# Products of constants between TensorE's first products, and one TensorE program in place of two, with the last outputs turned among the experts' first blocks

## What is computed

```python
def _attn_ref(r, k, v, w, a, b):          # (4, 8, 768, 40) each
    state = zeros((B, H, D, D))
    for t in range(S):
        y[:, :, t] = einsum('bhd,bhde->bhe', rt, state)
        Sa = einsum('bhde,bhe->bhd', state, at)
        state = state * wt[:, :, None, :] - einsum('bhd,bhe->bhde', Sa, bt) \
            + einsum('bhd,bhe->bhde', vt, kt)
...
x = y as (4, 768, 320)
x = _moe_ref(x)      # gates, the best 2 of 4 experts; each expert: causal softmax attention of width 64, then wo
return _moe2_ref(x)  # relu(x @ w_in), halves u and v, v normalised, w_spatial @ v + b, (u * v) @ w_out
```

## Time and profile before

| what | us |
|---|---|
| three executions | 980.12, 989.87, 990.72 |
| median | 989.87 |
| the profiled execution | 986.48 |
| its span, first to last instruction | 984.6 |
| TensorE busy in it | 946.3 (96%) |
| VectorE, ScalarE, GpSimd busy | 490.4, 450.4, 265.8 |
| mean granted TensorE clock | 0.977 of full |

### The profile page before, as it was taken

One profiled execution on the slowest core, in us unless ns is written; L12 is line 12 of the kernel. 1 busy time (PEld: TensorE's weight loads), 2 busy tenths in 40 slices (PEclk: granted clock), 3 DMA queues, 4 the chain that ended last, 5 costly groups with the idle time before them and its releaser, 6 DMA issues.

```text
span 984.6 us, 36043 instructions
## 1 busy us (share of the span) xinstructions
PE 946.3 (96%) x15444; PEld 685.4 (70%) x15444; DVE 490.4 (50%) x1395; ACT 450.4 (46%) x1074; POOL 265.8 (27%) x442
## 2 busy tenths in 40 slices
PE   7899999999999999999998999999999999999998
PEld 4788888888888888876655655566555665556555
DVE  7677777777777777754055244421434214342120
ACT  6456565565565655653237234342343423434501
POOL 7434645545545545522200001100011000110021
PEclk7589999999999999999999999999999999999999
DMA  4234434335333333241250000001000000000001
GB/s 153 64 82 131 111 99 111 102 95 151 105 95 111 104 92 113 73 121 30 60 203 1 2 0 1 1 28 54 0 1 2 27 14 0 1 2 27 14 0 41
DMA packets 37456, 59.68 MB, mean 61 GB/s; under 512 B 9137, under 2 KB 24305, under 8 KB 37297
## 3 DMA queue, kind: packets, MB, share of 16 engines
q1 hardware_dynamic: 37296, 57.37, 19.9%
HBM read 49.49 MB, written 7.86 MB: 58 GB/s over the span
## 4 chain that ended last, share of the span: by engine, by line
PE 85%; DVE 9%; issue 3%; ACT 2%; DMA 1%; DVEq 0%; POOL 0%; ACTq 0%; POOLq 0%
PE banks L1639 13%; PE banks L768 7%; PE banks L1578 5%; PE banks L1556 5%; PE banks L1590 4%; PE banks L1530 4%; PE banks L1607 4%; PE banks L1620 4%; PE banks L1651 4%; PE banks L701 4%; PE banks L956 4%; PE banks L968 3%; PE banks L946 3%; PE banks L829 3%; DVE state_z L1172 3%
## 5 line engine op out<-in xcount | busy, mean ns | idle before, releaser
L541 ACT ACTIVATE powers_z<-powers,parity 128x256 f32<-128x256 f32 x240 | 108.6, 500 | 157.2 <-DVE powers L1058 157.0
L1427 POOL TENSOR_TENSOR v_st<-v_st,u_t 128x384 f32<-128x384 f32 x32 | 31.9, 997 | 452.0 <-DVE v_st L1794 452.0
L1639 PE MATMUL banks<-w_st,v_n 128*128 128x384 f32 x384 | 139.0, 496 | 0.2 <-DVE v_n L1784 0.2
L768 PE MATMUL banks<-pq,powers_z 64*64 64x64 f32 (+1 forms) x3072 | 130.2, 228 | 2.0 <-ACT pq L533 1.5
L768 PEld LDWEIGHTS banks<-pq,powers_z 64*64 64x64 f32 x3072 | 112.7, 142 | 4.5 <-ACT powers_z L541 2.9
L1432 ACT ACTIVATE probs_t<-banks 128x512 f32<-128x512 f32 (+1 forms) x96 | 51.8, 543 | 121.2 <-PE banks L1578 121.1
L1639 PEld LDWEIGHTS banks<-w_st,v_n 128*128 128x128 f32 x384 | 67.5, 190 | 48.2 <-issue 10.8
L480 POOL TENSOR_TENSOR state<-state_sum,dc 128x160 f32<-128x160 f32 x92 | 56.9, 619 | 99.7 <-DVE state_sum L1160 99.7
L1737 DVE CUSTOM_DVE_ANT_0 probs<-banks,hide 128x128 f32<-128x128 f32 (+5 forms) x96 | 56.0, 622 | 51.6 <-PE banks L1556 51.1
L1152 DVE SCALAR_TENSOR_TENSOR vu_tok<-banks,minus,vz_tok 128x80 f32<-128x80 f32 x192 | 48.8, 296 | 64.7 <-PE banks L956 63.7
L1446 ACT ACTIVATE probs<-probs,neg_max 128x128 f32<-128x128 f32 (+5 forms) x96 | 63.3, 660 | 31.3 <-DVE neg_max L1737 31.3
(11 more groups left out here) (168 smaller groups left out, 1768.7 us busy)
## 6 DMA issues: line engine op xcount, KB each, us to landing
w_all<-decays_dram SPq DMA_DIRECT2D x48, 160.0 KB
w_all<-kb_ch_dram SPq DMA_DIRECT2D x48, 160.0 KB
vz_tok<-vz_tok_dram SPq DMA_DIRECT2D x24, 320.0 KB, 3.3
rz_ch<-rz_ch_dram SPq DMA_DIRECT2D x48, 160.0 KB
a_raw<-a_ch_dram SPq DMA_DIRECT2D x48, 80.0 KB
vc_tok<-vc_tok_dram SPq DMA_DIRECT2D x24, 160.0 KB, 2.6
x_dram<-y_ch SPq DMA_DIRECT2D x48, 80.0 KB
out_dram<-out_tok SPq DMA_DIRECT2D x24, 160.0 KB, 1.8
```

The source lines that it names most:

```text
L541: act.activation(powers_z[:, i, :, j, :], powers[:, i, :, :], ACT.Copy, scale=parity[:, j:j + 1])\
L768: ins = pe.matmul(to[r, k * n:k * n + n], powers_z[r, i, k, :, :].rearrange("p j t -> p (j t)"), right, start=True, stop=True)
L1639: ins = pe.matmul(bank[M_BANK + j % 2][:, 0:TH], v_n[:, i, d * P:d * P + P], w_st[:, i, t], start=(i == 0), stop=(i == BLOCKS - 1))
```

## The change

In the opening seven products of constants of 256 columns are added, and one of 256 becomes one of 512 columns: behind the warm-up, behind the two grams of unit 0, behind the turned keys, between levels 1 and 2 (the wider one), behind the grams of unit 1, behind level 3, and in the first two quarters of unit 0 between the first and the second hop.

At the end of the recurrence the turn of unit 23's outputs is taken out of the loop (`last_outputs`). The recurrence's TensorE program becomes a function that the second half's TensorE program calls first, so that there is one program and no branch between. `banks_done` loses the wait for the last outputs; `values_and_gates(0)` turns them behind its first two blocks, takes the blocks in the order `AFTER_OUTPUTS`, and waits for `y_taken` ahead of the block that writes bank 3 alone.

```diff
-        @block.tensor
-        def _(pe):
+        def tensor_program(pe):
...
+                if u == 0 and c < 2 and j == 0:
+
+                    warm(1, 256)
...
-                    if valid(u - 3):
+                    if valid(u - 3) and u - 3 < UNITS - 1:
...
+            def last_outputs():
+
+
+                pe.wait_ge(y_taken, at(UNITS - 2, y_taken))
+                turn_outputs(UNITS - 1)
+
 
             pe.wait_ge(consts, WARM_CONSTS)
             warm(4)
             pe.wait_ge(d_done, at(0, d_done))
             warm(1)
+            warm(1, 256)
 
 
             pe.wait_ge(kb_scaled, at(0, kb_scaled))
             first_grams(0)
             pe.wait_ge(n_read, at(0, n_read))
             grams(0, 1)
+            warm(1, 256)
             pe.wait_ge(akz_read, at(0, akz_read))
             level(0, 0)
             turn_keys(0)
+            warm(1, 256)
             level(0, 1)
-            warm(1, 256)
+            warm(1)
             level(0, 2)
             first_grams(1)
+            warm(1, 256)
             level(0, 3)
+            warm(1, 256)
             level(1, 0, 0, 4)
...
+            return last_outputs
...
-        shared.banks_done = ((y_taken, UNITS), (state_done, UNITS * NC), (oi_read, EP * FC))
+
+        shared.recurrence_on_tensor = tensor_program
+        shared.outputs_taken = (y_taken, UNITS)
+
+
+        shared.banks_done = ((state_done, UNITS * NC), (oi_read, EP * FC))
...
+        AFTER_OUTPUTS = (0, 2, 3, 4, 1, 5)
...
+            last_outputs = shared.recurrence_on_tensor(pe)
+
...
-                for j, i in enumerate(ORDER):
+
+                for step, j in enumerate(range(BLOCKS) if n > 0 else AFTER_OUTPUTS):
+                    i = ORDER[j]
...
+                    if n == 0 and step == 2:
+                        last_outputs()
+                    if n == 0 and V_BANKS[j] == 3:
+                        pe.wait_ge(*shared.outputs_taken)
```

## The result

| what | before | changed |
|---|---|---|
| executions, median | 987.41 (980.12 to 991.19) | 980.20 (973.86 to 986.86) |
| ratio, with its 95% interval | 1 | 0.9939 (0.9919 to 0.9959) |
| the profiled execution | 986.48 | 982.31 |
| its span | 984.6 | 980.5 |
| mean granted TensorE clock in it | 0.977 | 0.991 |

The change saves about 6 us of 987 by the ratio, 7.2 by the two medians. The time, 980.20, lies inside the range given (972 to 982) but outside that of the held clock (972.5 to 978). The saving is little more than half of the 11.5 us of the sum, and less than half of the 14.9 us between the forecast and the 989.87 that the kernel before was taken to need. By the ratio it belongs to "within 1%", which had a chance of 20%.

The account below looks back on a forecast made before the run. The prediction took TensorE to bound the kernel (946.3 us busy of a 984.6 us span). From the profiled 986.5 us it took 8.0 for the opening and 3.5 for the hand-over: 975.0 us, range 972 to 982.

Parts of the forecast that it names:

- the held clock: Likeliest case: the clock stays up in the opening and at the hand-over; 975.0 us, 972.5 to 978, chance 50%.
- the sum: Whole kernel: profiled execution 986.5 us less 8.0 for the opening and 3.5 for the hand-over gives 975.0.
- within 1%: Outcome class, not told from no change: the 985.5 case, the worse part of the 979 case, mixed executions; 20%.
- the prediction's own signs of being wrong: Clock falls in unit 0 in most executions, second level moves, or TensorE waits for VectorE's first copy behind the hand-over.
- the term for the opening: Up to unit 2: added products keep the clock up; 8.4 us gained less 0.4 for the products, net 8.0.
- The term for the hand-over: At 482 to 492 us: blocks around the last outputs' turn, 6.0 instead of 9.5 us, saving 3.5.
- The thin place in unit 0: Rival: clock still falls in unit 0's third quarter, where no product was added; 2.7 us back, 977.7 us; 22%.
- The clock holds only for a while: Rival: clock stays up past 13.6 us but falls among the levels; half of 8.0 lost, 979 us; 14%.
- Slower: Rival: clock stays low beyond 58 us, some 4 us per further unit; three units give 997 us; 3%.
- all of the low clock's time comes back: Rival: 44.4 us at half clock return 22.2, plus 1.9 of idle time at the hand-over; 962 us; 2%.
- faster by over 1%: Outcome class, below 980 us: the 975.0 and 977.7 cases, most of the 979 case, and the 962 case; 77%.
- the third case: Opening: clock stays up past 13.6 us, then falls among the levels of 64-wide products; 979 us; 14%.

Follow-up runs that it names:

- before_2: The kernel before, nothing changed, profiled a second time; one execution, 985.0 us.
- handover_only: The changed kernel without the added products, so the kernel before with only the new hand-over: 985.66 us, ratio 0.9970.
- fold_spread_before: The kernel before with the six loads of the folded weights issued one by one behind every second hop of unit 21: 985.74 us, ratio 0.9955.
- small_loads_before: The kernel before with loads of decays, keys, a, values and r moving a sixteenth of their data from unit 4 on: 981.87 us, ratio 0.997.
- more_instructions: The kernel before with its warm-up of four products of 512 constants made of eleven of 186: 988.62 us, ratio 0.9978.
- opening_only: The kernel before with all the opening's new products of constants and the old hand-over: 983.64 us, ratio 0.9948.
- changed_again: The changed kernel, nothing altered, timed and profiled a second time: 975.98 us, ratio 0.9905.
- fold_spread_2: The changed kernel with the six loads of the folded weights issued one by one in unit 21, timed again with more rounds: 975.37 us, ratio 0.9902.
- first_two_only: The changed kernel with only the two added products ahead of the first level kept in the opening: 980.43 us, ratio 0.9945.

## Why the prediction was wrong in size

**Up to unit 0 and at the hand-over the mechanism held, step by step.** The clock did not fall at 13.6; the second level stayed (17.81); the next step was 3.0 us, as 3.82 - 0.83 says; unit 0 started at 28.47 (forecast 28.3), unit 1 at 48.0, 47.0 and 46.5 in three profiles (forecast 46 to 47), unit 2 at 65.2, 64.3 and 63.2 (forecast 64); the hand-over took 5.83 (forecast 6.0) with no idle time, and VectorE's first copy waited for TensorE's own products alone. In unit 0 one of the prediction's own signs of being wrong came true: the clock fell there in six of eight profiles with the new opening.

**The step that failed is the one under "Sum":** the saving was worked out against one profiled execution, and that execution was taken as typical in the places where the change works. It was not. The starts of unit 2 over all profiles with the old opening (the kernel before, before_2, handover_only, fold_spread_before, small_loads_before) are 71.9, 71.5, 70.6, 64.8 and 67.0, mean 69.2 (more_instructions, whose warm-up is cut otherwise, has 72.5, with it 69.7); with the new one (eight profiles) 61.8 to 65.2, mean 63.7. So the term for the opening, 8.0 against its own execution (measured so: 6.7 to 8.7), is **5.4** against the mean, and opening_only measured 5.1. The mean of five starts that differ by 7 us has a standard error of 1.4 us, so 5.4 is a rough figure. In fold_spread_before the clock fell at 14.0 for 6.8 us and at 41.3 for 3.4; by chance the old opening can cost almost nothing (unit 2 at 64.8), and what a fix brings there is some 1 us. One price inside the term was too low as well: an added product of 256 columns, counted as 0.45 us, took 0.6 to 0.7 at the upper clock.

**The term for the hand-over**, 3.5, counted 1.5 us for a clock that falls. It was 3.69 against that profile. In four of the other five profiles of the old hand-over the clock did not fall there, and the difference is 2.26; the mean over all six is **2.8**, and handover_only measured 3.0. The idle time (2.05) was the sure part of this term and the clock an occasional one; the row at 484.6 showed it once, and once was taken for always.

5.4 + 2.8 = 8.2 us. The two halves alone measured 8.1, the pair with small loads 9.0. The three ratios of the changed kernel (0.9939, 0.9905, 0.9933) are 6.0, 9.4 and 6.6 us; the intervals of the last two hold 8.2, that of the first ends just below it, at 8.0. In the three groups that timed the changed kernel (35 executions of it, 56 of the kernel before) the means are 6.3, 9.9 and 5.7 us apart; together, each weighted by its precision, that is 7.2 us, 95% of it between 5.9 and 8.5. So 8.2 fits what was measured, at its upper end, and 11.5 does not.

**"Their spread is as large as what the opening's clock is worth, so I take it as different courses of the clock in the opening."** This was the second wrong step, and it let me forecast the profile's time less the sum, as if the 3.4 us between profile and median would come back. Most of the 3.4 was the luck of three executions: over twenty the median is 987.41, 0.9 above the profile. And the spread is only in part the opening's: with the old opening the start of unit 2 does differ by 7 us between profiles, but units 2 to 23 alone differ by 10 (408.3 to 418.4), in both kernels, and the changed kernel, whose opening is steadier (61.8 to 65.2), still ran from 973.9 to 986.9. The changed kernel came to 975 only where this section was short too (changed_again 411.5, no fall behind it: 976.1; fold_spread_2 408.3: 971.1).

**The rivals.** The thin place in unit 0, which had 22%, was the usual case (six of eight profiles), at 1.3 to 1.5 us instead of 2.7; the forecast counted it out of the likeliest time, though its own row spoke for it. "The clock holds only for a while" was what first_two_only did, not the change. "Slower" was nowhere to be seen. That all of the low clock's time comes back was as far off as said: the profile of before was low for 41.0 us up to unit 2 and the changed one for 6.8, half of the difference is 17.1, and unit 2 started 6.7 sooner. The page of the Trainium skill on this ("TensorE: Matmul & The Clock Gate", section on HAM oscillation) puts the penalty at the throttled time times one minus the ratio, which is the 17.1; these rows disagree with it. A step from level to level shrank from 3.82 to 3.00 us and not to 1.91: the 32 records of a level got shorter, the parts of the step on VectorE and ScalarE did not.

**Slips in the prediction's sums.** At the hand-over the idle time is 1.95 of 3.5 us, a little more than half and not two thirds. The bounds of the two terms (5.5 to 9.9 and 2.0 to 3.6) give 973.0 to 979.0, not 972.5 to 978. And 77% for "faster by over 1%" leaves 3 of the third case's 14, not most of it. None of these moves the forecast.

**Not foreseen at all:** the fall at 501 to 503, 2.84 us in two of three profiles. The sum assumed that nothing changes behind the hand-over. TensorE is busy for the same 2.08 us of 3.40 ahead of that place in both kernels, so the new hand-over does not bring it about by what TensorE does there; whether it does so by the time at which the place is reached (two of twelve in full, against none of six), or whether the six were too few, stays open. To prevent it cost 2.0 us in every execution, where it costs 2.84 in some.

## What to carry to other kernels

A stall of the clock that one profile shows at one place is an event with a frequency, not a cost: take two or three profiles of the same kernel before a term is sized by it, and price the sure part (idle time, work removed) apart from the part that comes and goes. Add products to hold a clock only where they stand in waits longer than themselves; in unit 0's last two quarters and among the scores they cost about what the falls cost. And where a kernel's executions scatter by 1%, compare sections of several traces before the scatter is given to a cause.

## What the runs showed of the hardware

In the stretch ahead of the first fall TensorE had no gap longer than 1.14 us and was busy 1.31 of 3.40; with two products more there (1.97 and 2.04 us) no fall followed at that place. The longest gap in the profile of before:

```profile
11.27 0.65 PE L718 MATMUL banks<-az_ch,kb_ch 128*32 128x64 f32 x32 [1.14 <-ACT az_ch L533]
```

At the lower level TensorE was busy for 88% of 30.7 us, mostly with products of 64 by 64, while the clock stayed down. Between executions of one kernel the course differs: low for 41.0 us and for 34.1 up to unit 2 and, with the same opening, for 10.2 (fold_spread_before, 14.0 for 6.8 and 41.3 for 3.4). Over 84 executions of the kernel before the time falls with the mean granted clock by 5.5 us for each 0.01 (a fitted line, correlation 0.66), over 35 of the changed one by 7.3 (0.85).

TensorE's program is itself a transfer: 16 KB for some 255 of its records, in the recurrence every 4.4 us on average (3.3 to 7.9), and about 1.0 us each (0.9 to 2.2). Beside data loads TensorE stops, often in the middle of a group of like products, for 0.2 to 2.5 us, 3.7 to 11.1 us in all between 60 and 470 us, the longest in before_2; with a sixteenth of the data moved there were 5 and 6 stops, 2.9 and 3.8 us in all.
